# Moving a scratch write, its read-back and the value scaling to other turns of the attention loop

## The reference

```python
# retention: attention with a decay in place of the softmax
scores = scale * np.matmul(q, k.transpose(0, 1, 3, 2))
gamma = 1.0 - 2.0 ** (-5.0 - np.arange(H, dtype=np.float32))
rel = pos[:, None] - pos[None, :]
Dmat = np.where(rel >= 0, gamma[:, None, None] ** rel[None, :, :], 0.0)
attn_out = np.matmul(scores * Dmat[None, :, :, :], v)
# 4 experts, 512 -> 1024 -> 512, weighted by normalized probabilities
p = domain_probs / (domain_probs.sum(-1, keepdims=True) + 1e-09)
for e in range(E):
    h = np.maximum(x @ w1[e], 0.0)
    out += p[:, e:e + 1] * (h @ w2[e])
# mish MLP, 512 -> 2048 -> 512
h = x @ w_in
out = (h * np.tanh(np.log1p(np.exp(h)))) @ w_out
```

## Time and profile before

| | us |
|---|---|
| median of 3 runs | 654.81 |
| lowest, highest | 651.81, 656.39 |
| the profiled execution's own time | 651.81 |
| its span in the profile | 650.0 |
| TensorE busy in it | 639.5 |

### The profile page before, as it was taken

One profiled execution on the slowest core, in us unless ns is written; L12 is line 12 of the kernel. 1 busy time (PEld: TensorE's weight loads), 2 busy tenths in 40 slices (PEclk: granted clock), 3 DMA queues, 4 the chain that ended last, 5 costly groups with the idle time before them and its releaser, 6 DMA issues.

```text
span 650.0 us, 10374 instructions
## 1 busy us (share of the span) xinstructions
PE 639.5 (98%) x4153; PEld 609.9 (94%) x4153; DVE 357.6 (55%) x624; ACT 220.6 (34%) x447; POOL 203.4 (31%) x167
## 2 busy tenths in 40 slices
PE   8899999999999999999999999999999999999998
PEld 5788999999999999999999999999998999999986
DVE  5757232423233332324232424349999999999772
ACT  3455212222212222212222212236464646555530
POOL 4654302222202222202212211224543545553220
PEclk9999999999999999999999999999999999999999
DMA  8955201111101111111211111111110111001001
GB/s 329 346 204 159 82 17 49 50 49 49 49 17 49 49 33 49 49 34 38 61 32 50 49 32 33 49 33 49 34 49 17 49 49 33 2 1 48 2 37 62
DMA packets 19312, 40.21 MB, mean 62 GB/s; under 512 B 2688, under 2 KB 3008, under 8 KB 19264
## 3 DMA queue, kind: packets, MB, share of 16 engines
q1 hardware_dynamic: 18448, 39.32, 18.9%
q10 hardware_dynamic: 816, 0.23, 0.2%
HBM read 37.17 MB, written 2.38 MB: 61 GB/s over the span
## 4 chain that ended last, share of the span: by engine, by line
PE 87%; DVE 9%; issue 2%; DMA 1%; ACT 1%; DVEq 0%; SPq 0%; ACTq 0%
PE bank L322 28%; PE bank L323 28%; PE bank L324 28%; PE bank L276 2%; DVE m_n L579 2%; DVE m_a L567 2%; PE bank L316 1%; DVE m_w L569 1%; DVE m_c L576 1%; DVE h_lo L511 1%; DMA qkv<-in_chunks 1%; DVE x_lo L558 1%; PE bank L280 0%; DVE acc_sb L553 0%; DVE qkv L490 0%
## 5 line engine op out<-in xcount | busy, mean ns | idle before, releaser
L225 POOL TENSOR_TENSOR w_lo<-w_raw,w_hi 128x512 fp32r<-128x512 f32 x96 | 128.5, 1339 | 301.8 <-ACT w_hi L219 301.7
L322 PE MATMUL bank<-x_hi,w_hi 128*128 128x384 f32 x576 | 194.7, 338 | 0.0
L324 PE MATMUL bank<-x_hi,w_lo 128*128 128x384 f32 x576 | 193.0, 335 | 0.0
L323 PE MATMUL bank<-x_lo,w_hi 128*128 128x384 f32 x576 | 192.7, 335 | 0.0
L428 ACT ACTIVATE h_hi<-h_act 128x384 fp32r<-128x384 f32 x144 | 75.6, 525 | 301.7 <-PE bank L324 266.9
L511 DVE TENSOR_TENSOR h_lo<-h_act,h_hi 128x384 fp32r<-128x384 f32 x144 | 83.2, 578 | 164.7 <-ACT h_hi L428 164.1
L322 PE MATMUL bank<-h_hi,w_hi 128*128 128x384 f32 x384 | 128.3, 334 | 0.1
L323 PE MATMUL bank<-h_lo,w_hi 128*128 128x384 f32 x384 | 128.3, 334 | 0.0
L324 PE MATMUL bank<-h_hi,w_lo 128*128 128x384 f32 x384 | 128.3, 334 | 0.0
L322 PEld LDWEIGHTS bank<-x_hi,w_hi 128*128 128x128 f32 x576 | 108.1, 188 | 2.9
L323 PEld LDWEIGHTS bank<-x_lo,w_hi 128*128 128x128 f32 x576 | 108.2, 188 | 1.7
(11 more groups left out here) (42 smaller groups left out, 495.9 us busy)
## 6 DMA issues: line engine op xcount, KB each, us to landing
w_raw<-in_weights SPq DMA_DIRECT2D x96, 256.0 KB, 2.6
qkv<-in_chunks SPq DMA_DIRECT2D x18, 512.0 KB, 7.1
pb<-probs_by_expert SPq DMA_DIRECT2D x3, 576.0 KB, 6.2
out<-acc_sb SPq DMA_DIRECT2D x2, 768.0 KB, 4.1
out<-acc_sb SPq DMA_DIRECT2D x3, 256.0 KB, 2.1
pb<-probs_by_expert SPq DMA_DIRECT2D x1, 384.0 KB, 5.4
pb<-probs_by_expert ACTq DMA_DIRECT2D x1, 192.0 KB, 6.3
consts<-in_consts SPq DMA_DIRECT2D x1, 146.0 KB, 4.8
```

Source lines behind the costliest of these rows:

```text
L225: pool.tensor_tensor(w_lo[:, part, u], w_raw[:, half % RAW], w_hi[:, part, u].bitcast(F32), ALU.subtract).then_inc(s_wl, 1)
L322: pe.matmul(out, w[0], x[0], start=first, stop=False)
L323: pe.matmul(out, w[0], x[1], start=False, stop=False)
L324: return pe.matmul(out, w[1], x[0], start=False, stop=last)
```

## The change

The scratch write, with its wait for the normalized probabilities, goes from ahead of ScalarE's loop into turn 0, behind state copy 0. The read-back of the first 384 tokens, with its wait for the write, goes from turn 5 to turn 2, behind the x_hi copy of chunk 1. GpSimd scales the values one chunk ahead of its turn and no longer two: `v_decay(1)` goes from ahead of the loop into turn 0, and each later one goes one turn back, so that `v_decay(7)` stands behind weight half 0's `unit_lo`, `v_decay(8)` behind half 1's, up to `v_decay(14)` behind half 7's.

```diff
-            act.wait_ge(s_pc, 4)
-            act.dma_start(probs_dram.rearrange("e (p j) -> p e j", p=P), p_norm[:, :, :]).then_inc(s_ps, 16)
             for c in range(TURNS + 1):
                 if c < CHUNKS and has_state(c):
                     state_copy(c)
                 if 0 < c <= CHUNKS:
                     act.wait_ge(s_xt, c)
                     act.activation(x_hi[:, :, CH * (c - 1):CH * c], x_tmp[:, (c - 1) % 2], ACT.Copy).then_inc(s_xh, 1)
-                if c == 5:
+                if c == 0:
+                    act.wait_ge(s_pc, 4)
+                    act.dma_start(probs_dram.rearrange("e (p j) -> p e j", p=P), p_norm[:, :, :]).then_inc(s_ps, 16)
+                if c == 2:
                     act.wait_ge(s_ps, 16)
                     act.dma_start(pb[:, 0, 0:TC], probs_dram[0, 0:TC].partition_broadcast(P)).then_inc(s_pb0, 16)
...
             pool.wait_ge(s_const, 16)
             v_decay(0)
-            v_decay(1)
             for c in range(CHUNKS + 1):
-                if c + 2 < CHUNKS:
-                    v_decay(c + 2)
+                if c + 1 < CHUNKS:
+                    v_decay(c + 1)
                 for half, turn in SPLIT_IN.items():
                     if turn == c:
                         unit_lo(pool, half)
```

## The result

The changed kernel takes 660.49 us (median of 11 runs, 657.13 to 662.88), the kernel before 654.06 beside it. The ratio is 1.0092 [1.0073, 1.0111], that is +6.0 us (4.8 to 7.3). The prediction said 660.0, +5.1, in a range of 655.5 to 664.8. The profiled execution took 659.61 (span 657.8), 7.8 over the one of before, and its mean granted clock was 0.992. The 12 recorded executions of the changed kernel have granted clocks of 1.0 (once, the fastest, 657.13), 0.997 (twice), 0.995 (six) and 0.992 (three). Rival 1 of the prediction, a clock that falls in the new gap, is what the profile shows.

A forecast was written before the change was run, and what follows sets the result against it. TensorE, busy 98%, was taken as the bound, with next to no idle time from turn 7 on. Turn 7 at +4.0 us with turn 14's +1.1 gave +5.1 on the median 654.81: 660.0 us, range 655.5 to 664.8.

The forecast's parts named there:

- Rival 1: TensorE's clock falls in the gap before turn 4, slowing one or two turns: +2.9 us, 662.9; chance 0.38.
- Part 1, the write's landing: Scratch write behind state copy 0: issued at 8.79, takes 9.6 us in full rings, lands at 18.4.
- Part 2, the wait: ScalarE waits from 13.84 in turn 2 for the write, holding state copy 3; turn 4 starts at 19.3, +4.9 us.
- What is won back in turns 4 to 6: Turns 4 to 6 take the undisturbed 1.77 us each, so 1.1 us of turn 4's delay is won back.
- the forecast's case: Write holds turn 4, v 7 holds turn 7, turn 14 halts, turns at 1.77 us: +5.1 us, 660.0; chance 0.42.
- the 2.0 taken off for turn 6: Turn 6 took 3.79 us before, instruction stall included, and is counted as 1.77: -2.0 us at turn 7.
- Part 3, turn 7: v 7, behind split 0, ends at 26.75 and holds turn 7: 2.2 us; alone +0.2 to +0.8.
- Part 3, turns 13 and 14: Scaling behind the splits: no halt at turn 13, margin 0.2; v 14 behind split 7 halts turn 14 by 1.1 us.
- The empty wait (2): Write lands within 5.0 us of issue, so ScalarE's wait is empty: +1.3 to +1.9 us, some 656.4; chance 0.10.
- the not slower (3): Empty wait, and TensorE's instructions come early enough to remove the 1.59 stall before turn 7: -0.1 us, 654.7; chance 0.04.
- Rival 4: Write lands at 19.3, nothing won back in turns 4 to 6, instruction stall delays v 7: +8.7 us, 663.5; chance 0.06.

The follow-up runs named there:

- the second look at that kernel: Kernel before with only the scaling of chunk 14 (v 14) moved behind weight half 7's split; unchanged up to turn 11; ratio 1.0036, +2.4 us.
- GpSimd's part: Kernel before with only GpSimd's scaling of v one chunk ahead instead of two, ScalarE as before; ratio 1.0030, +2.0 us.
- weight halves later: Kernel before with SP's loads reordered: chunks 6 and 7 ahead of weight half 0, the other halves behind later chunks; ratio 0.9995.
- ScalarE's part alone: Kernel before with only write and broadcast moved; ratio 1.0072, +4.7 us; executions in two groups, 654.35 to 656.49 and (upper) 658.25 to 660.30.

## Why the prediction was right, point by point

**Part 1, the write's landing.** Right in mechanism and size: 9.4 us for 9.6. It was issued at 8.12 and not at 8.79, while the first copy still ran. It was down at 17.5, 0.9 earlier than I had. That full rings are the cause was argued then and is shown now for the 3.3 us that two chunk loads fewer take off (6.1 us). The rest of the distance to the 4.0 us of the load at the start was not tested. The write alone shows no cost.

**Part 2, the wait.** Right: ScalarE idle 4.13 us, turn 4 +4.1 for +4.9; the difference is the earlier issue.

**What is won back in turns 4 to 6.** Here the forecast's case failed and rival 1 held. I had 1.1 us won back; the profile has 0.65 lost, since TensorE ran at 1.2 GHz from 16 to 22. Zeros in the gap bring the turns back to 1.8 us and the whole back by 2 us, so the clock's price is about 2 (rival 1 had 2.9), measured as the difference of two ratios whose intervals overlap by 0.0002, with six executions of the one. Its chance, 0.38, was too low: nine of the 12 executions were at 0.995 or below. But the kernel before isn't free of low clocks either: beside the experiments it was at 0.997 or lower in 69 of 91 executions, and the profiled one, at 1.0, was no typical one. Reading one profile at full clock, I took full clock for the norm. The same profile gave the term its size: turns 4 to 6 were slow in it (turn 6 at 19.02), while the second look at that kernel has turn 6 at 18.27 with turn 7 no earlier (22.89). So the 1.1 won back and part of the 2.0 taken off for turn 6 are a matter of one execution; what set turn 7 in both was the instruction stall's end.

**Part 3, turn 7.** The wait for v 7 is real, 2.49 for the 2.2 predicted, with the path named (x_hi 4, w_hi 0, split 0, v 7). Alone, though, it costs nothing, where I had +0.2 to +0.8: the instruction stall, 2.39 in that execution, covered it. The stall had been taken as a fixed 1.59, and in the second look at the kernel before it is 2.67.

**Part 3, turns 13 and 14.** Turn 14's halt is 1.07 for 1.1. Alone it costs 2.4, because a second stall follows it; the packets' times fit a request for instructions moved behind three large loads. In the whole change these loads come later than the packets, and only the halt is paid there.

**The sum.** +5.1 against +6.0 (4.8 to 7.3). It is within the interval, but composed differently: about 1 less at turn 4, about 2 more by the clock. These errors have opposite signs, so that the number came so near is in part luck: the case that it was worked out for, full clock, isn't the one that came. In the profiled execution, 4.1 at turn 4, +0.65 to turn 6, +0.45 at turn 7, +1.5 by the second fall of the clock and +1.3 from there to turn 14 make 8.0. That profile is set against one at full clock. Turn 7 takes 4.10 us in it, and 4.10 to 4.42 in four other profiles where an instruction stall and a low clock stand in the place of the wait for v 7 (GpSimd's part, the write's move, the broadcast's move, weight halves later), against 2.95 in the one of before. It is likely that the kernel before pays the same in its executions at 0.997 (59 of the 91, median 653.47; the 14 at 1.0 have 651.72), and that the second fall is therefore in the 7.8 of the two profiles and not in the 6.0 of the medians. No profile of that kernel at 0.997 shows it.

**The rivals.** The empty wait (2) and the not slower (3) are out: the wait was 4.13 us. Rival 2's case is what the lighter rings make of the changed kernel, 1.0023 where the rival had +1.3 to +1.9 us. Rival 4 didn't happen; no instruction stall shows in the changed kernel's profile. By the Trainium skill a DMA has a fixed cost of about 2 us ("DMA: Bandwidth & Descriptors", section "Anatomy of one DMA — SWDGE (gpsimd) path"), stated there for DMAs that GpSimd issues, while ScalarE issues this one. That is not what this small DMA takes beside full rings: 8.1 to 9.4 in the seven profiles that have it in turn 0 with the loads as they were, and 6.1 with two loads fewer.

**What stays open.** What sets the time of TensorE's instruction packets. They move with what TensorE does before (the broadcast's move and v 14 alone show that), but in the profiles neither reordering the loads nor thinning them rid the kernel of such stalls. And what the upper group of ScalarE's part alone does, beyond the lower clock, was caught in no profile. A candidate is a stretch at the lower clock ahead of turn 4: the write's move alone has one from 8 to 14 us, and both runs with zeros on the changed kernel have turns 2 and 3 at half pace. No experiment tested it.

## What to carry to other kernels

Before a DMA's wait is put into an in-order engine's stream, take its time from issue to landing at that place, in that load: 18 KB in 512 pieces took 9.4 us in full rings, and one wait for it held the state copy, TensorE, and then its clock. Then look at what stands behind a blocked instruction in every FIFO: a lead of one and not two put an operation whose data were there behind one whose data weren't. And read the granted clock of several executions before one profile is taken as the base.

## What the runs showed of the hardware that I had not expected

- The cost of a halt depends on what it moves: 1.26 us at turn 14 became 2.4 to 2.6, with an instruction packet that moved only behind most of 1.7 MB of broadcasts. Stalls with releaser "issue" of 0.8 to 2.7 us stand in nine of the twelve profiles of the experiments and in the one of before; in the changed kernel's there is none.
- The clock column can miss a slow stretch. In the profile with zeros before turn 4 it says 1.00 from 12 to 14, while the products there follow each other after 0.11 us for each pair; at full clock a pair takes 0.06:

```profile
12.00:14.00 2.00, 2.00 (x38) 1.93 (x36) 1.80 (x4) 0.76 (x3) 1.04 (x1) 1.00 1.05 398
```

```profile
12.66 0.31 PE L277 MATMUL bank<-qkv 64*64 64x64 f32 x1
12.70 0.31 PE L281 MATMUL bank<-qkv 64*64 64x64 f32 x1
12.77 0.31 PE L277 MATMUL bank<-qkv 64*64 64x64 f32 x1
```
